# Attention and two gated feed-forward layers on one core: the maxima of the local scores taken off by TensorE, and a new division of GpSimd's work

## The reference, cut to what matters

```python
# q, k, v: (4, 8, 576, 64)
# 1. pooled attention: q, k, v averaged over groups of 4 positions (576 -> 144)
out_d = sm_attn(q_d, k_d, v_d)                  # softmax(scale * q_d k_d^T) v_d
out_up = np.repeat(out_d, 4, axis=2)
# 2. local attention: mask = |i - j| < 4
scores = np.where(mask, scale * np.matmul(q, k.transpose(0, 1, 3, 2)), -1e9)
scores = scores - np.max(scores, axis=-1, keepdims=True)
attn = np.exp(scores); attn = attn / (attn.sum(-1) + 1e-9)
x = out_up + np.matmul(attn, v)                 # -> (2304 tokens, 512)
# 3. twice: x -> silu-gated feed-forward, 512 -> 2048 -> 512 (gates 1.0 and 1.702)
h = x @ w_in; g = h / (1 + np.exp(-gate * h)); x = g @ w_out
```

## Time and profile before

| | us |
|---|---|
| median of 3 runs | 808.96 (808.95 to 809.37) |
| profiled execution | 808.21 |
| its span, first to last instruction | 806.4 |
| TensorE busy in the span | 790.0 (98%) |
| VectorE busy | 646.0 (80%) |
| ScalarE busy | 530.8 (66%) |
| GpSimd busy | 208.8 (26%) |

### The profile page before, as it was taken

How to read it: one execution, slowest core, us unless ns; L and a number is a source line. 1 busy time by engine, 2 the same in 40 slices (tenths; PEclk the granted TensorE clock), 3 DMA queues, 4 the chain that set the end, 5 groups by cost and what they waited for, 6 DMA issues and landing times.

```text
span 806.4 us, 15771 instructions
## 1 busy us (share of the span) xinstructions
PE 790.0 (98%) x5864; PEld 763.4 (95%) x5864; DVE 646.0 (80%) x905; ACT 530.8 (66%) x849; POOL 208.8 (26%) x203
## 2 busy tenths in 40 slices
PE   9888799999999999999999999999999999999998
PEld 5666599999999999999999999999999999999998
DVE  7999899999898778998678898899555688456466
ACT  5878865677655678555687556678455786465673
POOL 5899977520274220445200000000000000000000
PEclk9999999999999999999999999999999999999999
DMA  8877647787878887677877778868887877878773
GB/s 282 266 249 238 197 150 259 262 298 233 283 236 268 260 315 245 217 261 258 289 267 249 239 250 262 256 224 272 306 275 257 273 249 266 304 250 271 264 256 136
DMA packets 100763, 205.51 MB, mean 255 GB/s; under 512 B 8784, under 2 KB 56400, under 8 KB 100688
## 3 DMA queue, kind: packets, MB, share of 16 engines
q1 hardware_dynamic: 100688, 204.51, 76.0%
HBM read 160.96 MB, written 43.52 MB: 254 GB/s over the span
## 4 chain that ended last, share of the span: by engine, by line
PE 88%; POOL 8%; issue 3%; DVE 1%; ACT 0%; POOLq 0%; DVEq 0%
PE hid L351 43%; PE yp L377 42%; POOL vpair L1038 2%; POOL vavg L1042 1%; PE yp L393 1%; POOL pband L1032 1%; POOL G L1062 1%; POOL G L1063 1%; POOL G L1068 1%; POOL G L1066 1%; POOL x L284 0%; DVE wh L315 0%; PE sc L1342 0%; PE hp L1342 0%; PE pt L1229 0%
## 5 line engine op out<-in xcount | busy, mean ns | idle before, releaser
L351 PE MATMUL hid<-xs,wh 128*128 128x384 f32 x2016 | 351.3, 334 | 0.7 <-issue 0.4
L351 PEld LDWEIGHTS hid<-xs,wh 128*128 128x128 f32 x2016 | 349.3, 188 | 1.7 <-issue 1.4
L377 PE MATMUL yp<-gr,wh 128*128 128x384 f32 x1968 | 342.1, 334 | 0.0
L377 PEld LDWEIGHTS yp<-gr,wh 128*128 128x128 f32 x1968 | 341.2, 188 | 0.1
L306 ACT ACTIVATE wh<-wr 128x1024 fp32r<-128x1024 f32 (+1 forms) x164 | 164.6, 1004 | 149.8 <-PE hid L351 120.0
L569 DVE TENSOR_TENSOR gr<-G,gr 128x768 fp32r<-128x768 f32 x144 | 137.9, 964 | 52.7 <-ACT gr L449 52.7
L449 ACT ACTIVATE gr<-G 128x768 fp32r<-128x768 f32 x144 | 121.8, 845 | 66.9 <-PE yp L377 66.8
L315 DVE TENSOR_TENSOR wh<-wr,wh 128x1024 fp32r<-128x1024 f32 x76 | 95.1, 1251 | 19.0 <-ACT wh L306 18.8
L412 ACT ACTIVATE G<-G 128x1152 f32<-128x1152 f32 x48 | 55.7, 1161 | 0.8 <-DVE G L564 0.8
L533 DVE TENSOR_TENSOR hv<-p,hid 128x384 f32<-128x384 f32 x48 | 26.3, 548 | 29.8 <-PE hid L351 28.0
L559 DVE TENSOR_TENSOR G<-hv,hid 128x384 f32<-128x384 f32 x48 | 26.3, 549 | 28.2 <-PE hid L351 28.2
(11 more groups left out here) (101 smaller groups left out, 748.0 us busy)
## 6 DMA issues: line engine op xcount, KB each, us to landing
wh<-rests SPq DMA_DIRECT2D x72, 512.0 KB, 3.7
wr<-sums_out SPq DMA_DIRECT2D x48, 512.0 KB, 4.7
wr<-in_w_out SPq DMA_DIRECT2D x36, 512.0 KB, 5.2
rests<-wh SPq DMA_DIRECT2D x36, 512.0 KB, 3.5
wr<-sums_in SPq DMA_DIRECT2D x40, 384.0 KB, 4.0
wr<-in_w_in SPq DMA_DIRECT2D x40, 256.0 KB, 3.5
qk<-in_qkT SPq DMA_DIRECT2D x11, 576.0 KB, 4.8
G<-in_w_in SPq DMA_DIRECT2D x12, 512.0 KB, 5.3
```

The costliest lines, as they stand in the source:

```text
L351: last = eng.matmul(hid[:, at, 0:HALF], lhsT=wh[:, w % SLOTS, part, a % 4, cc * P:(cc + 1) * P], rhs=xs[:, rest, q, cc, :], start=start an ...
L377: last = eng.matmul(yp[:, at + m, 0:HALF], lhsT=wh[:, w % SLOTS, part, p % 4, m * P:(m + 1) * P], rhs=gr[:, p, rest, :], start=start and p ...
```

## The change

The local scores no longer pass through VectorE's subtraction. VectorE takes the maxima as before, rounds them to fp32r (`mxr[:, 0]`) and forms the rest (`mxr[:, 1]`), 10 columns each. TensorE then adds four products to the scores in PSUM (`band_less`): minus the identity (`less`) times the rounded part and the rest, each repeated over the 64 columns of its window. ScalarE's exponentials read the scores in PSUM. The mask product of the next unit waits for the exponentials (`b_exp`), where it waited for the subtraction. On TensorE the pooled scores now stand right behind the local ones, and all four transposes before the new products; on ScalarE all four copies stand before the exponentials; on VectorE the sums of the next unit's q and k stand before the sums of the exponentials, except in unit 8.

GpSimd sums only 112 of the 144 groups of v in each unit (one row per partition, 256 and 128 columns wide where they were 512 and 256). The last 32 groups of four units together fill 128 partitions; they are loaded and summed four times in all, in units 0, 2, 4 and 7 (`LAST_SUMS`). The rests of x that attention prepares move from VectorE to GpSimd, B11 and B21 whole, T1, T3 and T2 in halves over two units each; the second half of T2 stands in unit 15. Two memsets of the buffers of v go.

```diff
-        def rest_x(eng, n, q):
+        def rest_x(eng, n, q, chunk=None):
             eng.wait_ge(self.x_hi, 7 * n + FILLS.index(q) + 1)
...
+            eng.tensor_tensor(xs[:, 1, q, at], features(n, q)[:, at], xs[:, 0, q, at].bitcast(F32),
+                              ALU.subtract).then_inc(self.x_lo if chunk != 0 else self.x_part, 1)
...
-    RESTS = {4: B11, 6: B21, 10: T1, 12: T3, 14: T2}
+    RESTS = {5: (B11, None), 6: (B21, None), 10: (T1, 0), 11: (T1, 1), 12: (T3, 0), 13: (T3, 1), 14: (T2, 0),
+             15: (T2, 1)}
+    LAST_SUMS = {0: 0, 2: 1, 4: 2, 7: 3}
+    LAST_LOADS = {1: 0, 3: 2, 5: 4}
...
 GpSimd, body:
+                if u.n in LAST_SUMS:
+                    at = LAST_SUMS[u.n]
+                    eng.wait_ge(last_in, DMA_INC * (at + 1))
+                    sum_groups(vn_last[:], vpair[:], vlast[:, at, :], summed(u.n) - 2)
...
+                sum_groups(vn[u.odd][0:MOST], vpair[0:MOST], vavg[u.odd][0:MOST], summed(u.n) - 1)
+                if u.n in RESTS:
+                    ffn.rest_x(eng, 0, *RESTS[u.n])
...
+            def sum_groups(groups, pair, to, done):
+                if done:
+                    eng.wait_ge(v_sum, done)
+                eng.tensor_tensor(pair, groups[:, 0:4 * D], groups[:, 4 * D:8 * D], ALU.add).then_inc(v_half, 1)
+                eng.wait_ge(v_half, done + 1)
+                eng.tensor_tensor(to, pair[:, 0:2 * D], pair[:, 2 * D:4 * D], ALU.add).then_inc(v_sum, 1)
...
 ScalarE, body:
-                    eng.activation(probs[u.odd], probs[u.odd], ACT.Exp, scale=scale_band).then_inc(b_exp, 1)
+                    eng.activation(probs[u.odd], scores.rearrange("p (b n) -> p b n", n=P), ACT.Exp,
+                                   scale=scale_band).then_inc(b_exp, 1)
...
 VectorE, body:
-                    eng.tensor_tensor(e, scores.rearrange("p (b s n) -> p b s n", s=2, n=WIN),
-                                      mxb[:].rearrange("p (b s) -> p b s", s=2).unsqueeze(3).broadcast_to(e.shape),
-                                      ALU.subtract).then_inc(b_sub, 1)
+                    eng.wait_ge(b_sub, u.n)
+                    eng.tensor_copy(mxr[:, 0], mxb[:]).then_inc(b_hi, 1)
+                    eng.wait_ge(b_hi, u.n + 1)
+                    eng.tensor_tensor(mxr[:, 1], mxb[:], mxr[:, 0].bitcast(F32), ALU.subtract).then_inc(b_lo, 1)
...
+                    if not last and not busy:
+                        sums(u.after())
                     eng.wait_ge(b_exp, u.n + 1)
...
                 elif n == UNITS:
                     ffn.rest_weights(eng, 1)
+                    eng.wait_ge(ffn.x_lo, 5)
                     ffn.rest_x(eng, 0, B22)
...
 TensorE:
-                eng.wait_ge(b_sub, u.n)
+                eng.wait_ge(b_exp, u.n)
...
+            def band_less(u):
+                eng.wait_ge(b_lo, u.n + 1)
+                for a in (0, HALF):
+                    for part in range(2):
+                        last = eng.matmul(scores[:, a * WIN:(a + HALF) * WIN], lhsT=less[:],
+                                          rhs=mxr[:, part, a:a + HALF].unsqueeze(2).broadcast_to([P, HALF, WIN]),
+                                          start=False, stop=part == 1, skip_group_check=True)
+                last.then_inc(b_sub, 1)
...
                     band_scores(u)
+                    avg_scores(u)
...
-                    for j in range(NLG):
+                    for j in range(NG):
                         group(old, j)
                 if last is not None:
-                    avg_scores(u)
+                    band_less(u)
```

More of the change, by code:

```diff
@@ L861, in build @@
             ident = sb("ident", [P, P])
+            less = sb("less", [P, P], F32R)
+            mxr = sb("mxr", [P, 2, NT], F32R)
             ident16 = sb("ident16", [P, P], BF16)
@@ L930, in build, with summed, pooled @@
         block = whole.enter_context(nc.Block())
+        def summed(n):
+            return n + 1 + sum(i <= n for i in LAST_SUMS)
+        def pooled(u, j):
+            at = u.n % 4 * REST
+            return (slice(0, MOST), slice(0, MOST)) if j == 0 else (slice(MOST, SD), slice(at, at + REST))
         def iterations(eng, start, body):
@@ L1084, in group @@
                 else:
-                    eng.activation(pta[:, j - NLG, :], src[:, 0:NA * AR], ACT.Copy).then_inc(p_cp, 1)
+                    rows = pooled(u, j - NLG)[1]
+                    eng.activation(pta[rows, j - NLG, :], src[rows, 0:NA * AR], ACT.Copy).then_inc(p_cp, 1)
             def body(u, first, last):
                 old = u.before()
-                if not first:
-                    for j in range(NLG):
+                if first:
+                    eng.wait_ge(consts, 3)
+                    eng.activation(less[:], ident[:], ACT.Copy, scale=-1.0).then_inc(less_cp, 1)
+                else:
+                    for j in range(NG):
                         group(old, j)
@@ L1183, in body @@
                     eng.reciprocal(rcb[:], smb[:]).then_inc(b_rcp, 1)
-                    if not last:
+                    if not last and busy:
                         sums(u.after())
@@ L1281, in group @@
                 else:
+                    keys, rows = pooled(u, j - NLG)
                     for c in range(NA):
-                        keys = (j - NLG) * REST
-                        last = transpose(to[:, c * AR:(c + 1) * AR], pavg[u.odd][:, c, keys:keys + P])
+                        last = transpose(to[0:rows.stop, c * AR:(c + 1) * AR],
+                                         pavg[u.odd][:, c, keys.start - rows.start:keys.stop])
                 last.then_inc(p_tr, 1)
@@ L1332, in body @@
                     eng.wait_ge(consts, 3)
-                if not first:
-                    for j in range(NLG, NG):
-                        group(old, j)
+                else:
                     band_product(old)
```

82 lines of the change are left out of this document (42 added, 40 removed).

## The result

The changed kernel takes 844.33 us (840.4 to 845.52, 4 runs), the kernel before 808.98 us in the same session (808.95 to 809.37): ratio 1.0427, 95% interval 1.0392 to 1.0463. It is 35 us slower where I had forecast 0.7, and far outside my range. Its profiled execution has a span of 843.3 us, 36.9 more than before, at a mean granted clock of 0.984 of full speed where it was 1.000.

What follows compares the result with a forecast made beforehand. VectorE paced attention's early units, with TensorE close behind and GpSimd at its limit later. Attention 2.4 us shorter, spent in the start and the T2 wait: +0.7 us, 809.7 us predicted; range 807.5 to 812.0.

Steps and rivals of the forecast that it cites:

- the two small operations: VectorE's two added 10-column operations per unit, between nothing and 0.22 us each; taken as 0.15 each.
- the pooled product: TensorE's last product in each unit, costed at 0.64 us from a row of the earlier profile.
- a little at each switch: Rival, chance 0.22: new products at 0.185 each plus switches between row counts make TensorE's turn 5.85; +2.5, 811.5 us.
- The four new products: TensorE's added fp32r products of 320 columns per unit: 0.62 us for four, between 0.53 and 0.74.
- The wait for T2: Passage to feed-forward: TensorE idles some 3 us for GpSimd's late rests of T2; rival that it hardly counts, chance 0.16.
- The start: Units 0 to 2: unit 3 starts at 22.7 against 21.40, a loss of 1.3 us.
- ScalarE's ring: Copies, exponentials and normalisation hide with 0.3 us to spare; rival that they do not, chance 0.12, +1.8, 810.8 us.
- GpSimd's turn: GpSimd's work per unit in units 10 to 14: 5.77 or 5.89 us, the slower engine there.
- where I had put a delay: Unit 8: VectorE's weight rest makes TensorE wait about 0.5 us for the pooled scores of unit 9.
- VectorE's relief: VectorE's need falls from 5.63 to about 5.1 us a unit, in all units but unit 8; it stops being the bound.

Runs made afterwards that it cites:

- GpSimd's part alone: Kernel before plus only GpSimd's halved sums of v and rests of x, VectorE still subtracting the maxima: 819.15 us; with pooled product grouped by row count 813.26.
- the repaired kernel: Changed kernel with the maxima in PSUM and the pooled product grouped by row count (112, 112, 32, 32): 815.26 us, ratio 1.0079.
- TensorE's part alone: Kernel before plus the four new products and new orders, maxima in PSUM; sums of v, pooled product and rests of x as before: 812.40 us, ratio 1.0044.
- the form with T2's rests on VectorE: Changed kernel with maxima in PSUM, pooled product grouped by row count, and T2's rests whole on VectorE in unit 14: 813.61 us, ratio 1.0057.
- the added copy: Kernel before plus a VectorE copy of the ten maxima from SBUF to an unused SBUF tile: 812.54 us, ratio 1.0044.
- the two-input maximum: Changed kernel with the maxima rounded by a two-input maximum of `mxb` with itself instead of a copy: 840.67 us; with grouped pooled product as well 837.61.
- kernel before with pauses: Kernel before with each GpSimd operation of attention waiting until the one ahead has ended: 811.19 us, ratio 1.0025.
- GpSimd's part alone, grouped, with pauses: Kernel before plus only GpSimd's changes, pooled product grouped by row count, each GpSimd operation of attention waiting for the one ahead to end: 818.42 us.

## Why the prediction was wrong

The forecast was 809.7 us and the time 844.33. Two terms of the sum carry 29.1 us of the difference, the two small operations and the pooled product; both are shown by the runs that repair them.

*The two small operations.* The step that failed is "No row shows these two; they lie between nothing and the 0.22 us that the reciprocal of 10 columns costs at most". They took up to 3.11 us, because VectorE's operands lie in SBUF while GpSimd works there. With `mxb` in PSUM they took 0.17 each, and the kernel gained 21.8 us, the largest of the terms. Most of it is found in three readings: TensorE's waits for `mxr` go from 9.3 to 0.7 us, the wait of 1.3 behind the weight rest goes, and the speed missing by the mean clock falls from (1 - 0.984) x 843.3 = 13.5 us to (1 - 0.997) x 820.5 = 2.5. So the lower clock costs about as much as the waits, an estimate of 11 against 9.9. It does not lie behind each wait: by the windows it followed the waits of 2.00 and 1.99 us for `mxr` (at 99.06 and 118.57) and the one of 1.31 for the sums, and not the one of 1.86 at 51.37. The prediction counted this sharing only where VectorE delays GpSimd (the 1.87 of the earlier trace rows) and never asked the opposite. The Trainium skill (SBUF — State Buffer, "SBUF: two separate sides"), which I cited there, says that the loser is blocked for the whole of the other's operation, and that either can be the loser. The trace agrees on the blocking and goes further: L1211, begun within one GpSimd operation, was blocked to its end and through the whole of three more.

*The pooled product.* "Local product 0.74 and pooled product 0.64" was taken over from the old form. It is 1.55, or 0.79 grouped: the step that failed is that costs of 128-row pieces were put on pieces of 112 and 32 rows. I had named the switches as a rival, "a little at each switch", with a turn of 5.85; the mechanism was right, and its size was off: 0.9 us a unit, a turn of 6.55. Grouping gave 7.2 us in the changed kernel and 5.9 in the one with GpSimd's part alone, and mixing cost 6.5 in the kernel before.

*The four new products.* 0.62 was too low: 0.73, at the upper bound of 0.74 that I took from the bf16 rows. With the old pooled product the turn is 5.67 where I had 5.61.

*The wait for T2.* Right in kind and near in size: 2.5 us in the changed kernel, 2.98 in the repaired one, for "some 3 us". I did not see that the clock would fall behind it: the twelve products that follow took 3.76 us to the next start (136.09 to 139.85) where I counted 2.1.

*The start.* Right in kind: from unit 0's mask product to unit 3's it is 1.57 us more than before (16.09) with TensorE's part alone, 1.77 in the repaired kernel; I had 1.3. In the changed kernel unit 3 starts at 25.79 instead of 22.7, so 3.1 late, 1.8 of it because the two pooled products done by then pay 0.9 each for the mixed rows.

*ScalarE's ring and GpSimd's turn.* Both held: no wait of TensorE on ScalarE's copies of `old` is left in the changed kernel, and in the halved sums of v the second stands 0.80 us behind the first and takes 0.48 (0.81 and 0.43 forecast). GpSimd's terms add up to 5.80 or 5.92 us and not to the 5.77 or 5.89 that I wrote; that moves the forecast by 0.15. With both repairs TensorE turns in 5.8 but for units 8 and 9, and GpSimd keeps up, busy for 9.77 of 10 us from 80 to 90 us. In those two units TensorE waits 0.50 and 0.66 us for GpSimd; it is about where I had put a delay, but the two turns are 1.5 us longer together instead of 0.5.

*What VectorE's relief is worth.* The pace in the early units passed to TensorE, whose own sequence grew to the old turn. In the later ones GpSimd sets it with TensorE's part alone (9.7 of 10 us busy), TensorE in the repaired kernel (9.93 of 10 from 70 to 90 us). There the twelve turns from unit 3 to unit 15 are 0.91 us shorter than before (70.94 instead of 71.85), so the gain exists and is small. It is lost at the two ends: of the 6.08 us by which that kernel (815.26) resumes late, unit 3 is late by 1.88, and the last unit and the passage take 5.11 more, of which 2.98 is the wait for T2 and 1.9 the twelve products behind it at the lower clock (4.01 us where 12 of the 18 in the earlier trace rows take 2.13). Against the kernel before, the form with T2's rests on VectorE (813.61) resumes 5.85 us late, of which unit 3 is late by 1.71, the twelve turns by 0.39, and the last unit and the passage by 3.75, where the rest of T2 is held up.

Open is why VectorE gets in at the end of one GpSimd operation in the kernel before and of four in the changed one, when no pause lies between them in either. That a pause ends the hold-up is shown; that only a pause does is contradicted by the added copy. Open too is what decides whether the clock falls behind a wait of 1.3 to 1.9 us.

## What to carry to other kernels

Before a small operation is put on VectorE in TensorE's path, look at where its operands lie and what GpSimd does at that moment: its price can be that of GpSimd's run of operations, not its own, and with an operand in PSUM it kept its 0.17 us. When matmuls with few rows are split off, group them by row count; the rows before and after look alike, and only the distance from start to start shows the price. And a wait of TensorE of about 2 us is often paid twice: read the granted clock in the windows behind it before trusting any sum.

## What the runs showed of the hardware

- A VectorE operation of 10 columns with its operands in SBUF took up to 3.11 us beside four GpSimd operations in a row and 3.69 beside five, instead of 0.17, one of 1024 columns 3.09 to 3.29 instead of 1.21, one of 768 columns 2.79 instead of 0.95. With a pause behind each GpSimd operation the one of 10 columns waited for one at most (1.70 us). With its first operand in PSUM it took 0.17 in all 16 units.
- Pieces of two fp32 matmuls of 144 columns follow each other at 0.39 us when their row counts alternate (112 or 128 with 32), at 0.16 in one form.
- Behind nearly every wait of TensorE of 2.0 us and more in attention the granted clock fell (0.53 in the window from 120 to 130 us of the changed kernel); the exception is a wait of 2.47 with the two-input maximum, at 132.92. Behind shorter waits it fell in some places and not in others: it fell behind 1.31 us (changed kernel, at 71.75), 1.70 (kernel before with pauses, at 71.61) and 1.74 (GpSimd's part alone, grouped, with pauses, at 60.73), and stayed full behind 1.86 (changed kernel, at 51.37) and behind the three waits of 1.47 of the kernel before, which showed full speed in every window of 10 us from 20 to 120 us.
